# Splitting the 144 down-sampled keys as 112 + 32 (four units together), loading raw weights in chunks, and re-timing the side work of GpSimd, ScalarE and VectorE

## The reference, cut to what matters

```
# attention: q, k, v are 4 x 8 x 576 x 64
q_d, k_d, v_d = mean over groups of 4 positions (576 -> 144)
out_d   = softmax(scale * q_d @ k_d.T) @ v_d          # 144 queries, 144 keys
out_up  = repeat(out_d, 4, axis=2)
scores  = scale * q @ k.T, masked to |i - j| < 4
out_local = softmax(scores) @ v
x = out_up + out_local                                 # 2304 tokens x 512
# first MLP, d_ff 2048
h = x @ w_in;  x = (h - tanh(h)) @ w_out
# second MLP, d_ff 1536
out = (sigmoid(x @ w_gate) * (x @ w_val)) @ w_out
```

## Time and profile before

| | |
|---|---|
| median of 3 runs | 898.12 us (897.77 to 899.66) |
| the profiled execution's own time | 898.21 us |
| its span | 896.4 us |
| TensorE / VectorE / ScalarE / GpSimd busy | 98% / 65% / 43% / 32% of the span |
| granted TensorE clock | 1.00 |
| bytes moved | 197.01 MB, mean 220 GB/s |

### The profile page before, as it was taken

One profiled execution on the slowest core, in us unless ns is written; L12 is line 12 of the kernel. 1 busy time (PEld: TensorE's weight loads), 2 busy tenths in 40 slices (PEclk: granted clock), 3 DMA queues, 4 the chain that ended last, 5 costly groups with the idle time before them and its releaser, 6 DMA issues.

```text
span 896.4 us, 15665 instructions
## 1 busy us (share of the span) xinstructions
PE 881.3 (98%) x6088; PEld 829.9 (93%) x6088; DVE 580.5 (65%) x922; ACT 381.2 (43%) x720; POOL 286.6 (32%) x237
## 2 busy tenths in 40 slices
PE   7998999999999999999999999999999999999998
PEld 5877899999999999999999999999999999999997
DVE  8999876578756668565679656576444466444445
ACT  4777855455333344233354544453222243222221
POOL 5889776591030001030136558513100001000000
PEclk9999999999999999999999999999999999999999
DMA  8875497669554545455315777788755555755511
GB/s 259 248 232 159 178 350 275 239 228 403 186 207 171 212 141 213 168 187 201 118 48 209 283 282 282 281 337 320 281 212 211 212 211 211 262 231 211 211 48 70
DMA packets 36137, 197.01 MB, mean 220 GB/s; under 512 B 3712, under 2 KB 5248, under 8 KB 23008
## 3 DMA queue, kind: packets, MB, share of 16 engines
q1 hardware_dynamic: 29584, 162.16, 48.6%
q0 software_dynamic: 4032, 29.36, 8.7%
q10 hardware_dynamic: 2448, 4.49, 1.7%
HBM read 139.90 MB, written 56.10 MB: 219 GB/s over the span
## 4 chain that ended last, share of the span: by engine, by line
PE 92%; POOL 4%; DVE 2%; issue 1%; ACT 1%; DMA 0%; ACTq 0%; POOLq 0%; DVEq 0%
PE banks L848 48%; PE banks L920 22%; PE banks L1036 17%; PE banks L822 1%; PE banks L794 1%; POOL prob L589 1%; PE banks L779 1%; POOL v_four L582 1%; PE banks L768 1%; PE banks L839 1%; PE banks L811 1%; POOL win L629 0%; POOL prob_d L589 0%; POOL v_down L586 0%; DMA qk<-in_k_dram 0%
## 5 line engine op out<-in xcount | busy, mean ns | idle before, releaser
L848 PE MATMUL banks<-x_op,pair 128*128 128x384 f32 x1512 | 276.1, 335 | 0.0
L848 PEld LDWEIGHTS banks<-x_op,pair 128*128 128x128 f32 x1512 | 265.2, 188 | 7.2
L920 PE MATMUL banks<-g_parts,mid 128*128 128x384 f32 x1152 | 226.3, 335 | 1.4 <-DVE x_all L1498 1.3
L920 PEld LDWEIGHTS banks<-g_parts,mid 128*128 128x128 f32 x1152 | 201.7, 188 | 3.1 <-DVE x_all L1498 3.1
L848 PE MATMUL banks<-x_op,win 128*128 128x384 f32 x1008 | 201.4, 335 | 0.0
L848 PEld LDWEIGHTS banks<-x_op,win 128*128 128x128 f32 x1008 | 176.7, 188 | 0.8 <-issue 0.7
L1036 PE MATMUL banks<-wout,p_parts 128*128 128x512 f32 x648 | 162.9, 393 | 0.0
L1498 DVE TENSOR_TENSOR x_all<-banks,x_all 128x384 f32<-128x384 f32 x168 | 92.8, 555 | 83.8 <-PE banks L920 83.3
L1036 PEld LDWEIGHTS banks<-wout,p_parts 128*128 128x128 f32 x648 | 120.4, 188 | 20.7
L1624 DVE TENSOR_TENSOR x_all<-banks,x_all 128x512 f32<-128x512 f32 x90 | 62.1, 690 | 112.3 <-PE banks L1036 112.3
L648 POOL DMA_DIRECT2D wout<-kept_out x12 | 6.4, 537 | 211.4 <-PE banks L1036 211.4
(11 more groups left out here) (98 smaller groups left out, 985.5 us busy)
## 6 DMA issues: line engine op xcount, KB each, us to landing
pair<-kept_pair SPq DMA_DIRECT2D x24, 1792.0 KB, 10.5
win<-kept_in SPq DMA_DIRECT2D x16, 1792.0 KB, 7.5
kept_pair<-pair SPq DMA_DIRECT2D x12, 1792.0 KB, 11.7
mid<-kept_mid POOLq DMA_DIRECT2D x16, 1024.0 KB, 5.1
kept_in<-win SPq DMA_DIRECT2D x8, 1792.0 KB, 7.2
wout<-kept_out POOLq DMA_DIRECT2D x12, 1024.0 KB, 11.6
kept_mid<-mid SPq DMA_DIRECT2D x8, 1024.0 KB, 5.1
kept_out<-wout SPq DMA_DIRECT2D x6, 1024.0 KB, 15.0
```

What stands on the lines that cost most here:

```text
L848: mm = pe.matmul(bk[:, 0:T], weights[:, w, p - 1, kk, :], x_op[:, p - 1, x, kk, :], start=(first and kk == 0 and a == 0), stop=(last and k ...
L920: mm = pe.matmul(bk[:, 0:T], w[:, wp, f, m * P:(m + 1) * P], g[:, gp, 2 * f + t, :], start=(f == 0 and a == 0), stop=(f == 1 and a == 2))
```

## The change

Down-sampled keys are now split as 112 (`MOST`) and 32 (`FEW`). A unit's own tile has 112 keys, `[MOST, FACTOR, P]`. The remaining 32 keys of four units k*4 to k*4+3 share one tile `v_few` of 128 partitions, loaded by one 256 KB DMA (four in all) at u = 0, 1, 3 and 7 behind `load_v(u)`, each waiting for `s_few`, and summed by GpSimd once per four units in two instructions (`few_pairs`, `few_fours`). `down_values` contracts over 112 keys and over 32 keys at partitions 0, 32, 64 or 96; `turn_rest` transposes, in its second half, the last 32, 64, 96 or 128 keys, depending on u % 4. The zeroing of `v_four` goes. The first two raw weights are loaded as two DMAs of 256 KB each at u = 1, 2 and 9, 10. GpSimd's side work is one piece a period from t = 1 to 16, and takes over the low parts of products 1 and 7 from VectorE. ScalarE's `half_weight_high(0)` comes two periods earlier and both halves of `half_weight_high(1)` stand at t = 16. Cut to the lines spoken of:

```diff
-    FEW = SD - P
+    FEW = P // 4
+    MOST = SD - FEW
...
+        def rows_of(u, c):
+            return slice(0, MOST) if c == 0 else slice(u % 4 * FEW, u % 4 * FEW + FEW)
...
-            def load_v_few(u):
-                wait(sp, s_vd, u - 1)
+            def load_v_few(k):
+                wait(sp, s_few, 2 * k)
...
-            sp.wait_ge(s_four, 2)
-            load_v_few(0)
             for u in range(UNITS):
-                if u + 1 < UNITS:
-                    load_v_few(u + 1)
                 if u + 3 < UNITS:
                     load_qk(u + 3)
                 load_v(u)
-                if u == 2:
-                    load_raw(0)
-                if u == 8:
-                    load_raw(1)
+                if u in (0, 1, 3, 7):
+                    load_v_few((0, 1, 3, 7).index(u))
+                if 1 <= u < 3:
+                    load_first_raw(0, u - 1)
+                if 9 <= u < 11:
+                    load_first_raw(1, u - 9)
...
             def value_sums(u):
-                pool.tensor_tensor(four[:, :, 0:2, :], four[:, :, 0:2, :], four[:, :, 2:4, :], ALU.add).then_inc(s_vd_step, 1)
+                pool.tensor_tensor(four[:, 0:2, :], four[:, 0:2, :], four[:, 2:4, :], ALU.add).then_inc(s_vd_step, 1)
...
-                pool.tensor_tensor(v_down[u % 2][:, :, :], four[:, :, 0, :], four[:, :, 1, :], ALU.add).then_inc(s_vd, 1)
+                pool.tensor_tensor(v_down[u % 2][:, :], four[:, 0, :], four[:, 1, :], ALU.add).then_inc(s_vd, 1)
+            def few_pairs(k):
+                pool.wait_ge(s_vfew, 16 * (k + 1))
+                pool.tensor_tensor(v_few[:, 0:2, :], v_few[:, 0:2, :], v_few[:, 2:4, :], ALU.add).then_inc(s_few, 1)
+            def few_fours(k):
+                wait(pool, s_vald, 4 * (k - 1))
+                pool.wait_ge(s_few, 2 * k + 1)
+                pool.tensor_tensor(v_few_down[k % 2][:, :], v_few[:, 0, :], v_few[:, 1, :], ALU.add).then_inc(s_few, 1)
...
+                if t < 3:
+                    few_sums(t - 1)
+                if 3 <= t < 5:
+                    weight_sums(0, ((0, 1), (2, 3))[t - 3])
                 if t == 5:
-                    weight_sums(0, (0, 1))
+                    few_pairs(2)
+                if 6 <= t < 10:
+                    first_weight_low(t - 6)
                 if t == 6:
-                    weight_sums(0, (2, 3))
-                if t == 8:
-                    first_weight_low(0)
-                    first_weight_low(1)
+                    few_fours(2)
                 if t == 9:
-                    first_weight_low(2)
-                    first_weight_low(3)
+                    few_pairs(3)
                 if 10 <= t < 13:
                     x_sums(0, (t - 10,))
                 if t == 13:
+                    few_fours(3)
                     weight_sums(1, (0, 1))
-                if t == 14:
+                if 14 <= t < 16:
+                    first_x_low((1, 7)[t - 14])
+                if t == 16:
                     weight_sums(1, (2, 3))
             x_last_sum(0)
...
             def down_values(u):
                 pe.wait_ge(s_vd, u + 1)
+                pe.wait_ge(s_few, 2 * (u // 4 + 1))
...
-                if 7 <= t < 9:
-                    half_weight_high(0, t - 7)
+                if 5 <= t < 7:
+                    half_weight_high(0, t - 5)
...
-                if t == 15:
-                    half_weight_high(1, 0)
                 if t == UNITS:
                     x_high(0, 3)
                 if 1 <= t <= UNITS:
                     copy_local(t - 1, 0)
                     copy_local(t - 1, 1)
                 if t == UNITS:
+                    half_weight_high(1, 0)
                     half_weight_high(1, 1)
                     copy_c(0, C22)
                     copy_c(0, C21)
...
-            for i in range(2):
-                dve.memset(v_four[i][:, 1, :, :], 0.0).then_inc(s_four, 1)
...
-                if 13 <= t < 15:
-                    x_low(0, (1, 7)[t - 13])
                 if t == UNITS:
+                    dve.wait_ge(s_xlo, 2)
                     x_low(0, 6)
```

More of the change, by code:

```diff
@@ L191, in attention_and_mlps @@
         early = Room(RING + 2 * WIN_BYTES, RING + 2 * WIN_BYTES + 4 * WS)
-        v_four = [room.tile(f"v_four{i}", [P, 2, FACTOR, P]) for i, room in enumerate((low, early))]
-        v_down = [low.tile(f"v_down{i}", [P, 2, P]) for i in range(2)]
+        v_four = [room.tile(f"v_four{i}", [MOST, FACTOR, P]) for i, room in enumerate((low, early))]
+        v_down = [low.tile(f"v_down{i}", [MOST, P]) for i in range(2)]
+        v_few = low.tile("v_few", [P, FACTOR, P])
+        v_few_down = [low.tile(f"v_few_down{i}", [P, P]) for i in range(2)]
         prob_d = [room.tile(f"prob_d{i}", [DROWS, 3, SD]) for i, room in enumerate((low, low, early))]
@@ L223, in attention_and_mlps @@
         s_zeros = sem("zeros_ready")
-        s_four = sem("v_four_cleared")
+        s_vfew = sem("v_few_loaded")
+        s_few = sem("v_few_sums")
         s_band = sem("band_ready")
@@ L579, in value_sums, with few_sums @@
             def value_sums(u):
-                pool.wait_ge(s_v4[u % 2], 32 * (u // 2 + 1))
+                pool.wait_ge(s_v4[u % 2], 16 * (u // 2 + 1))
                 four = v_four[u % 2]
-                pool.tensor_tensor(four[:, :, 0:2, :], four[:, :, 0:2, :], four[:, :, 2:4, :], ALU.add).then_inc(s_vd_step, 1)
+                pool.tensor_tensor(four[:, 0:2, :], four[:, 0:2, :], four[:, 2:4, :], ALU.add).then_inc(s_vd_step, 1)
                 wait(pool, s_vald, u - 1)
                 pool.wait_ge(s_vd_step, u + 1)
-                pool.tensor_tensor(v_down[u % 2][:, :, :], four[:, :, 0, :], four[:, :, 1, :], ALU.add).then_inc(s_vd, 1)
+                pool.tensor_tensor(v_down[u % 2][:, :], four[:, 0, :], four[:, 1, :], ALU.add).then_inc(s_vd, 1)
+            def few_sums(k):
+                few_pairs(k)
+                few_fours(k)
+            def few_pairs(k):
[5 more added lines that the diff above has]
+                pool.tensor_tensor(v_few_down[k % 2][:, :], v_few[:, 0, :], v_few[:, 1, :], ALU.add).then_inc(s_few, 1)
             def scale_rows(view, inv, n, width):
@@ L600, in weight_sums @@
                 if su < Q1:
[L601 removed]
+                    pool.wait_ge(s_raw[su % 3], raws(su))
                 else:
@@ L627, in first_weight_low @@
                 part = slice(piece * WS // 4, (piece + 1) * WS // 4)
-                pool.wait_ge(s_whi, highs(0))
+                pool.wait_ge(s_whi, highs(0) - 1 if piece < 2 else highs(0))
                 pool.tensor_tensor(dst[:, 1, :, :, :].rearrange("p o k n -> p (o k n)")[:, part], raw[:, :, :].rearrange("p o n -> p (o n)")[:, part],
@@ L671, in x_sums, with first_x_low @@
                         pool.tensor_tensor(tmp[:, 1, :, :], b22, b12, ALU.subtract).then_inc(s_t, 1)
+            def first_x_low(p):
+                pool.wait_ge(s_xhi, splits(0, p))
+                pool.tensor_tensor(x_op[:, p - 1, 1, :, :], x_source(0, p), x_op[:, p - 1, 0, :, :].bitcast(F32),
+                                   ALU.subtract).then_inc(s_xlo, 1)
             def x_last_sum(s):
@@ L1102, in copy_rest @@
                 wait(act, s_vald, u - 1)
-                rows = slice(0, ROWS[hh].stop)
+                rows = slice(0, max(HALF, rows_of(u, hh).stop))
                 act.activation(prob_tr[u % 2][rows, hh, :], bank[B_R[hh]][rows, 0:REST], ACT.Copy).then_inc(s_cr, 1)
```

23 lines of the change are left out of this document (13 added, 10 removed).

## The result

The changed kernel took 900.53 us (median of 20 runs, 899.33 to 902.40); the kernel before, 899.01 in 20 runs beside it (897.77 to 900.03). Ratio 1.0019, interval 1.0013 to 1.0025: about 1.7 us slower, where 4.4 us faster was forecast, and outside the range of 892.0 to 896.3.

What follows compares the result with a forecast made beforehand. GpSimd was taken to set the pace in periods 8 to 16, with TensorE the bound otherwise. -5.9 + 0.6 + 0.85 + 0.05 = -4.4 us gave 893.7 us, from 892.9 to 894.6 (chance 0.60).

Steps and rivals of the forecast that it cites:

- Periods 8 to 16: Attention from 51.68 to 101.38 us: 43.8 instead of 49.70 us, -5.9, as GpSimd no longer sets the pace.
- TensorE's mode changes: One further gap of about 0.20 us in `turn_rest` at u = 4, 8, 12: +0.6 us, between 0 and 6.0.
- The tail: After the last attention periods: +0.85 us from ScalarE's added half, +0.05 from GpSimd's weight sums beside VectorE's `x_low`.
- The half on ScalarE: Added half of `half_weight_high(1)` between `copy_local(15)` and `copy_c`, delaying C22, C21 and product 5: +0.85 us.
- rival 2: Start and tail take more: `v_few` late (+1), VectorE and GpSimd excluding each other in period 16 (+1): 895.7 us; chance 0.14.
- The start: First periods: same bytes loaded, `v_few` landing at about 13 to 15.5 and 21.1 to 23.5 us; cost 0 to 1.5, taken 0.
- the slack of `prob`: At the start, TensorE needs `prob` 1.75 us after GpSimd's usual end, so a late `v_few` costs 0 to 1.5 us.
- Rival 4: Slower: TensorE pays two further mode changes in every unit, 6.0 us instead of 0.6: 899.1 us; chance 0.05.
- Period 16's `turn_local` near 96: Sign of being right: period 16 starts near 96 us, after `turn_local` every 5.5 us.
- the gap before the 112*32 form: Sign of being right: TensorE shows a gap of about 0.2 us before the 112*32 form in `turn_rest`.
- product 5 about 0.85 us later: Sign of being right, in the tail: product 5 starts about 0.85 us later against `turn_local(15)`.
- waits on `v_few`: Sign of being wrong: waits for the shared 32-key loads show in the profile; no size given.

## Why the prediction was wrong, point by point

- **Periods 8 to 16: right in kind, and in size partly by luck.** Forecast -5.9 + 0.6 = -5.3, measured -5.40 (44.30 for 49.70). Two errors cancel: the +0.6 did not come, and seven periods took 38.70 us instead of 38.2, since GpSimd waited 0.85 and 0.65 us for late `v_four` and TensorE lost 0.45 us to it in period 12. The value sums were as forecast: 0.88 and 0.41 us to the next start where 0.86 and 0.40 were said. But the account of what wins was too narrow. With the large sums and the side work spread, the same periods took 45.49, 4.2 less than before; with the small sums and the side work as before, 47.40 and 46.83, 2.3 and 2.9 less, and nothing of that in periods 8 and 9, where GpSimd waited for ScalarE. So the spread brings most of it.
- **TensorE's mode changes: +0.6 forecast, 0 seen.** Weight loads of the changed kernel, period 13 (unit 12, a multiple of 4):

```profile
90.01 0.11 PEld L845 LDWEIGHTS banks<-ident,prob 72*72 72x72 f32 x1
90.11 0.26 PEld L850 LDWEIGHTS banks<-ident,prob_d 112*32 112x32 f32 x3
90.55 1.01 PEld L860 LDWEIGHTS banks<-prob_tl,v_win 70*64 70x64 f32 x32 [0.18 <-issue]
```

  No gap stands before the 112*32 form; the 0.18 behind it is that of the earlier trace rows. By the Trainium skill (TensorEngine Tiling (Array Packing), Key Properties) a change of mode drains; the switch from 72*72 shows no such price here, before 80, 64 or 32 columns.
- **The tail: +0.9 forecast, +1.90 measured**, just beyond the bound that was given (0.85 and up to 1 more). The half on ScalarE was right in kind (0.85); the collision of `weight_sums(1, (2, 3))` with `x_low` was priced at 0.05, and some 1 us is left for it, as rival 2 had it: 0.53 of it is ScalarE's wait for GpSimd. The two were not tested apart; with both moved the tail was 6.94.
- **The start: 0 forecast, bound 1.5, measured +7.45 in the profiled execution.** This is the step that failed. Its sentence "the bytes are the same" was true, and the landing of 4.9 to 7.3 us was taken from loads of other shapes: 16 contiguous rows, and a raw weight. That put the first landing at 13 to 15.5 us and the second at 21.1 to 23.5; the loads of this shape took 10.5 and 7.1 us and landed at 19.0 and 27.5. Three things lay behind it:
  1. *The shape*, shown: four loads with the same bytes cut the waits from 7.3 to 2.3 us and gave 3.7 us at the start of period 8 (2.8 with the old side work, where the median fell by 4.2); two of outermost size 2 cost 7.8 us more at the median.
  2. *The order on GpSimd*, a chain that could be read from the code: `few_sums` stands ahead of the next `normalise`. I costed the lateness at the slack of `prob` (1.75 us) and then took nothing from it, since GpSimd would catch up. It can't where TensorE waits for `prob` in the same period.
  3. *The clock and stops of TensorE*: every version with the split that was profiled had a stretch below 0.9 or a period of 7 us or more in the first 60 us, while the kernel before and the first weight's side work alone had none. The side work alone, without the split, had one too (0.54 in 12 to 18 us), so the split is not shown to be its cause. What stays after the four loads, 3 to 4 us at the start of period 8, is of this kind, and in the change with four loads also waits for `v_four`; how much is which was not taken apart. In 20 to 80 us the DMA engines were also busier for the same rate: a share of 0.75 at 228 GB/s before, 0.78 at 231 with the first weight's side work alone, 0.82 and 0.98 at 231 in the two kernels with four loads (split alone, change), 0.86 at 224 in the change. Shares of 8 rows for `v_four` did not lower it (0.98 at 233); the cause was not found.
- **Rival 4**, slower, had the right sign for a reason that did not exist. No rival was the start itself: the bound of 1.5 us on a load of a shape that no row showed was too narrow, and 0.87 for faster too sure.
- **What the profile would show.** Period 16's `turn_local` near 96 was wrong (103.43), and so were the gap before the 112*32 form (none) and product 5 about 0.85 us later (1.48). One wait for `prob` after period 8 was left (0.45). Periods of 5.5 us held from period 4 on but for 12, and the value sums and ScalarE's two halves in a row were right; "waits on `v_few`", named as a sign of error, is what came.

Still open: why the split's loads land later even as four, what stops TensorE in mid-sequence, and what lowers the clock in the slower half of the runs of before.

## What to carry to other kernels

Before you merge small loads into one, look at the outermost size of its source and destination: a 256 KB load with outermost size 4 took 10.5 and 7.1 us, while as four loads the same bytes were there 7.5 and 5.6 us after the first was issued, and the engine whose list holds the wait passes it on to everybody. When an engine is the bound in some periods only, spread its side work first, and see that the piece it is given does not wait for another engine's: that alone won 3.5 us here, without touching the layout of the data; of the loads only the raw weights' moved. Price a load in a saturated stretch by a row of the same shape in that stretch; with none, leave a wide bound.

## What the runs showed of the hardware that was not expected

- A load of the same 256 KB took 10.5 and 7.1 us as one with outermost size 4, and 2.2 to 8.0 (median 5.5) as four with 32 rows.
- Stops of TensorE of 1.58 to 2.53 us between instructions of one sequence, with nothing to wait for by the profile, where the DMA engines were at 0.97 to 1.05. That late instructions are the cause (the profile lists instruction traffic among the DMA queues) was only argued, and a high share is not enough: the change with four loads had 1.01 to 1.03 from 54 to 72 us with TensorE busy all the time.
- The granted clock was lower behind most of the stops, but not all. Behind the stop of 1.58 us it was 0.69 and 0.74 in the next two windows of 6 us, and the two periods took 5.1 us more than two usual ones; the period with the stop of 2.53 us took 4.3 more, at 0.86 and 0.85; that with the stop of 1.93 us took 2.2 more, at 1.00.
- GpSimd's sums of 256 elements took 1.45, 1.33 and 1.44 us beside VectorE's `x_low`, and 0.72 alone. The Trainium skill (SBUF — State Buffer, SBUF: two separate sides) has a VectorE instruction with two inputs in SBUF and a GpSimd instruction that reads SBUF exclude each other for a whole instruction; the traces agree.
